# From attention to the first mixing step: where ScalarE's first casts and VectorE's last reciprocals stand, and the receptance input of step 0 in four pieces

## What is computed

```python
xk = mu_k * x + (1 - mu_k) * x_prev
xr = mu_r * x + (1 - mu_r) * x_prev
k  = max(xk @ w_k, 0)
y  = sigmoid(xr @ w_r) * (k * k @ w_v)
```

## Time and profile before

| what | value |
|---|---|
| time, median of 3 runs | 770.95 us (769.91 to 771.16) |
| the profiled execution's own time | 772.05 us |
| its span in the profile | 770.3 us |
| TensorE busy with matmuls | 741.0 us, 96% of the span |
| VectorE (DVE) busy | 494.1 us, 64% |
| ScalarE (ACT) busy | 357.5 us, 46% |
| GpSimd (POOL) busy | 182.9 us, 24% |
| mean granted TensorE clock | 0.991 of full speed |

### The profile page before, as it was taken

How to read it: one execution, slowest core, us unless ns; L and a number is a source line. 1 busy time by engine, 2 the same in 40 slices (tenths; PEclk the granted TensorE clock), 3 DMA queues, 4 the chain that set the end, 5 groups by cost and what they waited for, 6 DMA issues and landing times.

```text
span 770.3 us, 13475 instructions
## 1 busy us (share of the span) xinstructions
PE 741.0 (96%) x4054; PEld 661.7 (86%) x4055; DVE 494.1 (64%) x905; ACT 357.5 (46%) x702; POOL 182.9 (24%) x215
## 2 busy tenths in 40 slices
PE   5999999998999999999999999999999999999994
PEld 4888888886989999999999998788888788888882
DVE  8899999996586856859487797622223745453261
ACT  4687877875652606244251432222124644353250
POOL 3345455453200000000020000223323232323231
PEclk9999999998999999999999999999999999999997
DMA  5667676551000010100101071167110176441000
GB/s 158 212 202 224 195 228 190 165 159 43 24 1 1 0 42 1 42 1 1 42 1 43 3 270 42 43 246 274 41 32 27 41 257 235 143 144 40 20 22 8
DMA packets 43063, 74.41 MB, mean 97 GB/s; under 512 B 10061, under 2 KB 20470, under 8 KB 43012
## 3 DMA queue, kind: packets, MB, share of 16 engines
q1 hardware_dynamic: 38676, 64.30, 25.3%
q0 software_dynamic: 4336, 9.47, 3.6%
HBM read 65.31 MB, written 10.57 MB: 99 GB/s over the span
## 4 chain that ended last, share of the span: by engine, by line
PE 83%; DVE 10%; issue 2%; ACT 2%; DMA 1%; ACTq 0%; POOL 0%; POOLq 0%; DVEq 0%
PE ps L841 20%; PE ps L842 20%; PE ps L843 20%; PE ps L779 3%; PE ps L707 2%; PE ps L999 2%; PE ps L733 2%; PE ps L732 2%; PE ps L831 2%; DVE negm L1380 2%; PE ps L710 2%; PE ps L774 1%; DVE sig L1564 1%; PE ps L753 1%; PE ps L908 1%
## 5 line engine op out<-in xcount | busy, mean ns | idle before, releaser
L841 PE MATMUL ps<-we_hi,hT_hi 128*128 (+1 forms) x176 | 73.4, 417 | 2.1 <-DVE o_sb L1856 1.4
L841 PE MATMUL ps<-we_hi,xgT_hi 128*128 (+1 forms) x176 | 70.6, 401 | 0.2 <-DVE xgT_lo L1755 0.2
L1317 ACT ACTIVATE hT_hi<-ps 128x512 fp32r<-128x512 f32 x44 | 26.1, 597 | 94.5 <-PE ps L999 49.4
L842 PE MATMUL ps<-we_lo,xgT_hi 128*128 (+1 forms) x176 | 69.7, 396 | 0.0
L843 PE MATMUL ps<-we_hi,xgT_lo 128*128 (+1 forms) x176 | 69.7, 396 | 0.0
L842 PE MATMUL ps<-we_lo,hT_hi 128*128 (+1 forms) x176 | 69.5, 395 | 0.0
L843 PE MATMUL ps<-we_hi,hT_lo 128*128 (+1 forms) x176 | 69.4, 394 | 0.0
L1151 ACT ACTIVATE pT<-ps 128x256 f32<-128x256 f32 (+2 forms) x192 | 63.1, 388 | 9.3 <-PE ps L733 8.9
L841 PE MATMUL ps<-xm_k_hi,wk_hi 128*128 128x384 f32 x192 | 65.2, 339 | 2.0 <-DVE ksq L1543 1.7
L841 PE MATMUL ps<-ksq_hi,wv_hi 128*128 128x384 f32 x192 | 66.0, 344 | 0.9 <-DVE yT L1578 0.9
L531 POOL TENSOR_TENSOR hi<-qk_raw,hi 64x576 fp32r<-64x576 f32 x32 | 45.2, 1412 | 85.8 <-DVE aug L1407 85.8
(11 more groups left out here) (277 smaller groups left out, 1835.4 us busy)
## 6 DMA issues: line engine op xcount, KB each, us to landing
we_raw<-w SPq DMA_DIRECT2D x12, 2048.0 KB, 11.8
qk_raw<-qkT SPq DMA_DIRECT2D x32, 576.0 KB, 3.9
v_sb<-v SPq DMA_DIRECT2D x16, 320.0 KB, 4.9
inv<-inv_scratch SPq DMA_DIRECT2D x32, 144.0 KB, 4.3
y_scratch<-ytok SPq DMA_DIRECT2D x6, 768.0 KB, 3.5
wk_raw<-w_k SPq DMA_DIRECT2D x8, 256.0 KB, 4.5
wv_raw<-w_v SPq DMA_DIRECT2D x8, 256.0 KB, 4.9
wr_raw<-w_r SPq DMA_DIRECT2D x4, 256.0 KB, 4.8
```

What stands on the lines that cost most here:

```text
L841: mm(dst, a_hi, b_hi, start=(k == 0), stop=False)
L842: mm(dst, a_hi, b_lo, start=False, stop=False)
L1317: nc.scalar.activation(hT_hi[:, half * FC // 2:(half + 1) * FC // 2, :].rearrange("p f t -> p (f t)"), ps[:, 3 + half, :], ACT.Copy).then_ ...
```

## The change

- ScalarE: the casts of chunks 0 and 1 (`xm0_hi`) move from behind `copy_out(29, 0)`, ahead of head 30's exponentials, to behind those exponentials. Those of chunks 2 and 3 stay behind head 31's.
- VectorE: `xm0_lo` of chunks 0 and 1 moves ahead of `invert(29)` in round 30. `invert(30)` moves from ahead of `sum_xm` of chunks 2 and 3 to behind `xm0_lo` of chunk 3.
- Step 0's receptance input is split in four pieces: `xmr_hi(f - 1)` on ScalarE behind the square's cast, and `xmr_lo(f - 1)` on VectorE behind the square's low part, for f = 1 to 4, in place of one cast and one subtraction of four times the size at f = 4.

```diff
+            def xmr_hi(c):
+                act.wait_ge(xm_summed, DC + c + 1)
+                nc.scalar.activation(xm[1][0][:, c, :], xsum[1][:, c, :],
+                                     ACT.Copy).then_inc(xm0_is_hi if c < DC - 1 else xm_is_hi, 1)
...
                 if i + NBUF < NHEAD:
                     cast_tops(i + NBUF)
+                if i >= NHEAD - 2:
+                    for c in range(2):
+                        xm0_hi(c + (i == NHEAD - 1) * 2)
                 if WFIRST <= i < NHEAD - 1:
                     split_wm_hi(i - WFIRST)
-                if i == NHEAD - 1:
-                    for c in range(2, DC):
-                        xm0_hi(c)
                 copy_out(i, 0)
-                if i == NHEAD - 3:
-                    for c in range(2):
-                        xm0_hi(c)
...
-                    if s == 0 and f == DC:
-                        xm_hi(0, 1)
                     act.wait_ge(relu_done, k + 1)
                     nc.scalar.activation(ksq_hi[:, f, :], relu_k[:, f % 2, :], ACT.Square).then_inc(ksq_is_hi, 1)
+                    if s == 0 and 1 <= f <= DC:
+                        xmr_hi(f - 1)
...
+            def xmr_lo(c):
+                if c < DC - 1:
+                    dve.wait_ge(xm0_is_hi, DC + c + 1)
+                else:
+                    dve.wait_ge(xm_is_hi, 1)
+                last = vec.tensor_tensor(xm[1][1][:, c, :], xsum[1][:, c, :], xm[1][0][:, c, :].bitcast(F32), ALU.subtract)
+                if c == DC - 1:
+                    last.then_inc(xm_split, 1)
...
-                if i:
+                if i == NHEAD - 2:
+                    for c in range(2):
+                        xm0_lo(c)
+                if 0 < i < NHEAD - 1:
                     invert(i - 1)
...
-                if i == NHEAD - 2:
-                    for c in range(2):
-                        xm0_lo(c)
             for c in range(2, DC):
                 xm0_lo(c)
+            invert(NHEAD - 2)
...
                     if s == 0 and f == 1:
                         invert(NHEAD - 1)
-                    if s == 0 and f == DC:
-                        xm_lo(0, 1)
+                    if s == 0 and 1 <= f <= DC:
+                        xmr_lo(f - 1)
```

## The result

| | before | changed |
|---|---|---|
| time, median | 770.95 us (769.91 to 771.69, 5 runs) | 765.77 us (765.16 to 766.95, 5 runs) |
| the profiled execution's own time | 772.05 us | 765.25 us |
| its span | 770.3 us | 763.5 us |
| mean granted clock | 0.991 | 0.997 |

The ratio is 0.9937, 95% interval 0.9922 to 0.9952: faster, by 5.2 us in the medians and by 6.8 us between the two profiled executions. The forecast was 6.7 us and 764.2; the range of 763.0 to 767.6 holds the result, but its core of 763.2 to 765.0 doesn't. The two differences are not the same thing, and most of what follows is about the 1.6 us between them.

What follows compares the result with a forecast made beforehand. TensorE was taken as the bound, so only its waits and low clock could be won. Step 0's start, -5.35 us, and its gap, -1.35, gave -6.7 us: 764.2 us from 770.95, range 763.0 to 767.6.

Steps and rivals of the forecast that it cites:

- What bounds the kernel: Whole kernel: TensorE's matmuls cover 741.0 of 770.3 us, so only its waits or low clock can be won.
- Part 1: Head 30, casts behind the exponentials: `head_pv(30)` starts at 184.83, not 187.12; next scores at 187.65, not 192.56; 4.9 us.
- The block takes 2.82, not 5.44 us: Head 30's last 14 matmuls, at full clock in place of the half clock behind the 2.22 us gap.
- Part 2: Head 31, reciprocal last: step 0 starts at 192.3 for 197.64, a gain of 5.35 us, low parts 0.6 us ahead.
- Part 3: Step 0, four pieces: gap ahead of f = 7 falls from 1.70 to 0.5 us; f = 7 at 207.4 for 214.14.
- Behind it: From f = 7 on: old order, the 0.93 us wait for yT moves along, and nothing takes the gain back.
- The clock falls all the same: Rival, near heads 30 and 31: short TensorE gaps drop the clock to 1.2 GHz, losing 3.3 us; 767.5 us; chance 0.12.
- The pieces bring nothing: Rival, step 0: VectorE is full, the 1.7 us gap stays at f = 6 or 7; 765.6 us; chance 0.12.
- The other two: Rivals: old waits only handed on in the heads, 770.5 us, 0.03; half clock in step 0, slower, 772.3 us, 0.03.

Runs made afterwards that it cites:

- the filled gap: The kernel before with ten matmuls, whose output nobody reads, in TensorE's gap in head 30: 769.63 us against 771.46, ratio 0.9982.

## Why the prediction was right, and where it was off

**What bounds the kernel**: right. All that was won came out of TensorE's gaps and clock.

**Part 1**: the mechanism was right in each step: `copy_out(29, 1)` at 182.49 (said 182.58), the next wait the row copy with 0.55 us (0.6), `head_pv(30)` at 184.78 (184.83), clock 1.00, `load_row(31)` hidden. The term that was mis-sized is "The block takes 2.82, not 5.44 us", with the slow scores ahead of it. It is true of that one execution. The price of the half clock behind this gap is 0 to 3.2 us by execution, in five traces 0, 1.7, 1.7, 1.7 and 3.2, and some 1.8 us in the median by the filled gap. I charged the largest, which by the mean clocks comes in about one execution of ten. The profiled execution took 772.05 us, more than any of the five timed beside it; the text noticed the 1.1 us over the median and carried them over as a constant, where it was part of what the change removes.

With 2.1 us of waits (13.21 to 11.07 in A), 1.3 us in B and 1.8 us of clock the sum is 5.2 us. The medians show 5.2 us, and 4.6 us the other time (771.75 to 767.19). The two profiled executions differ by 6.8 us, nearly as forecast, because the one of before had the long fall.

**Part 2**: right. Step 0 started at 192.21 (192.3); the casts and low parts were done 0.7 us ahead (0.6). Alone, the reciprocal's move is worth 0.5 us in the trace and nothing that the medians can tell; behind the casts' move it is worth 0.4 us (A 11.49 to 11.09).

**Part 3**: right, and close: multiply at 203.98 (203.9), two sums in 1.85 us, gap of 0.40 us (0.5), f = 7 at 207.42 (207.4). The lock told of beside it is borne out: with the multiply elsewhere the sums of f = 4 take 0.75 us, and those of f = 5, where it then falls, take 1.66. The pieces themselves were never held there, and VectorE, though full, kept up.

**Behind it**: right; the wait for yT is 0.9 us as before.

**The rivals**: none came true. "The clock falls all the same" did not come in any of the nine traces without the long idle gap, five of which have one of about 0.5 us there. "The pieces bring nothing" is refuted by B. The other two never came near. The range held because it was drawn out to the first two rivals; that the median of 765.77 stands next to the second rival's 765.6 is chance, since another term than that rival's was short. The argument for the first rival, that a fall had happened in this place, took one trace for a property of the program.

## What to carry to other kernels

A profile is one execution. Where a term of the sum hangs on the granted clock, take a second trace of the same kernel, compare the mean clock of all its timed executions, or price the term from nothing to its full size; here the idle gap came every time, the half clock behind it did not. And when an engine is freed from a wait, look in the same row for the next thing on the list: here the row copy behind two sums, which cost nothing to put ahead of them since GpSimd's multiply held the sums anyway.

## What the hardware did that I had not expected

A gap of 2.1 to 2.2 us on TensorE in the same place of the same work led to 6.7, 3.5 or no us at the 1.2 GHz level. Ten matmuls that filled it (2.44 us) took 1.8 us off the median. The first heads differ too, 1.73 or 2.99 us for the same eight matmuls at 18.4 us, and with such differences in the first 28 us, which no kernel here touched, everything behind them moves by up to 1.4 us. Why an execution has one or the other was not tested.
